# Two changes to the order of VectorE's work in a fused kernel: routing steps moved by a place, weight splits gathered in one tile

## What is computed

```python
logits = x @ w_gate                                  # first layer adds noise, then takes the best two
expert_idx = np.argmax(logits, axis=1)               # second layer: the best one
gate_w = probs[np.arange(N), expert_idx]
for e in range(E):
    xe = x[expert_idx == e]
    out[expert_idx == e] = gate_w * (np.maximum(xe @ w1[e], 0.0) @ w2[e])
```

## Time and profile before

| | us |
|---|---|
| median of 3 runs | 1131.98 |
| lowest and highest | 1128.28 and 1138.9 |
| the profiled execution | 1126.27 |
| its span, first to last instruction | 1124.5 |

### The profile page before, as it was taken

One profiled execution on the slowest core, in us unless ns is written; L12 is line 12 of the kernel. 1 busy time (PEld: TensorE's weight loads), 2 busy tenths in 40 slices (PEclk: granted clock), 3 DMA queues, 4 the chain that ended last, 5 costly groups with the idle time before them and its releaser, 6 DMA issues.

```text
span 1124.5 us, 30641 instructions
## 1 busy us (share of the span) xinstructions
PE 1067.7 (95%) x7894; PEld 998.0 (89%) x7895; DVE 796.0 (71%) x1432; ACT 572.1 (51%) x1233; POOL 488.3 (43%) x530
## 2 busy tenths in 40 slices
PE   3999899999999999999999999999999899999995
PEld 3779799889999899999999899998998888999995
DVE  8998999999588655456566775556678875666652
ACT  2345345545634434455666344446765555655542
POOL 1000455556445444444455344444445544545452
PEclk9998899999999999999999999999999999999998
DMA  8439332342342232445554332335964644543510
GB/s 262 124 106 263 92 117 81 109 120 99 94 115 77 87 98 78 138 148 172 164 154 141 96 92 90 96 108 174 273 200 145 156 113 120 158 130 109 154 44 14
DMA packets 105111, 143.77 MB, mean 128 GB/s; under 512 B 27818, under 2 KB 82413, under 8 KB 104812
## 3 DMA queue, kind: packets, MB, share of 16 engines
q1 hardware_dynamic: 85612, 99.74, 30.5%
q0 software_dynamic: 19456, 43.53, 13.3%
HBM read 111.53 MB, written 35.09 MB: 130 GB/s over the span
## 4 chain that ended last, share of the span: by engine, by line
PE 70%; DVE 12%; issue 8%; DMA 3%; DVEq 2%; ACT 2%; SPq 1%; POOL 0%; ACTq 0%; POOLq 0%
PE ps_y L1937 18%; PE ps_y L1943 9%; PE ps_h L1874 7%; PE ps_h L1878 6%; PE ps_h L1881 6%; PE ps_h L1875 6%; PE ps_h L1862 4%; PE ps_h L1694 3%; DVE h_lo L1086 2%; PE ps_x L1852 2%; PE ps_y L1964 2%; PE ps_x L1851 2%; DVE prod L959 1%; DMA row<-in_moe_w_dram 1%; DVE prod L729 1%
## 5 line engine op out<-in xcount | busy, mean ns | idle before, releaser
L1937 PE MATMUL ps_y<-w_hl,h_hi 128*128 128x400 f32 (+1 forms) x1344 | 370.4, 360 | 2.6 <-DVE y L1106 1.8
L1086 DVE SCALAR_TENSOR_TENSOR h_lo<-ps_h,h_hi 128x512 fp32r<-128x512 f32 x404 | 258.7, 684 | 152.8 <-ACT h_hi L1525 112.4
L598 POOL DMA_INDIRECT row<-x_rows,read_now x200 | 229.3, 1146 | 277.1 <-issue 234.1
L1525 ACT ACTIVATE h_hi<-ps_h 128x512 fp32r<-128x512 f32 x370 | 202.7, 596 | 224.4 <-PE ps_h L1862 137.4
L1943 PE MATMUL ps_y<-w_hl,h_lo 128*128 128x200 f32 (+1 forms) x1344 | 293.5, 259 | 1.1 <-DVE h_lo L1086 1.0
L1937 PEld LDWEIGHTS ps_y<-w_hl,h_hi 128*128 128x128 f32 x1344 | 244.6, 188 | 3.5 <-issue 2.4
L1943 PEld LDWEIGHTS ps_y<-w_hl,h_lo 128*128 128x128 f32 x1344 | 235.6, 191 | 2.1 <-DVE h_lo L1086 2.0
L1874 PE MATMUL ps_h<-xa_hi,w1a_hi 128*128 128x256 f32 x672 | 203.2, 302 | 3.7 <-issue 1.3
L1878 PE MATMUL ps_h<-xa_lo,w1a_hi 128*128 128x256 f32 x672 | 191.1, 284 | 2.8 <-DVE xa_lo L1068 2.6
L1875 PE MATMUL ps_h<-xa_hi,w1a_lo 128*128 128x256 f32 x672 | 189.3, 282 | 0.0
L1881 PE MATMUL ps_h<-xb_hh,w1b_hl 128*128 128x256 f32 x672 | 188.6, 281 | 0.0
(11 more groups left out here) (245 smaller groups left out, 1630.3 us busy)
## 6 DMA issues: line engine op xcount, KB each, us to landing
w_raw<-in_moe_w_dram SPq DMA_DIRECT2D x32, 768.0 KB
w1a_raw<-in_moe_w_dram SPq DMA_DIRECT2D x32, 512.0 KB
w1b_raw<-in_moe_w_dram SPq DMA_DIRECT2D x64, 256.0 KB
x_rows<-tok SPq DMA_DIRECT2D x14, 512.0 KB, 3.3
x_rows<-tok SPq DMA_DIRECT2D x28, 256.0 KB
x_pad<-in_x_dram SPq DMA_DIRECT2D x2, 2688.0 KB, 10.4
row<-x_rows,read_now POOLq DMA_INDIRECT x200
x_pad<-y_rows SPq DMA_DIRECT2D x14, 200.0 KB
```

The source lines that it names most:

```text
L598: pool.indirect_dma_start(out=row[:, buffer, u, 0:XW if p < C else SCALED_W], out_offset=None, in_=x_rows[p], in_offset=bass.IndirectOffse ...
L1086: nc.vector.scalar_tensor_tensor(out=h_lo[:, i * GF:(i + 1) * GF, :], in0=ps_h[:, i, :].rearrange("p (f t) -> p f t", f=GF), scalar=0.0, i ...
L1525: act.activation(h_hi[:, i * GF:(i + 1) * GF, :], ps_h[:, i, :].rearrange("p (f t) -> p f t", f=GF), ACT.Relu).then_inc(h_hi_ready, 1)
L1937: nc.tensor.matmul(first, h_hi[:, i, cols], both_w, start=(i == 0), stop=False)
```

## The change

Two things. In the passes of the second layer (p >= 2) VectorE takes all three low parts of the next expert in the tile in which it takes w1a, and SyncE of the third pass issues all three loads in the expert's first tile. And in the second and third pass routing steps stand elsewhere: `choose_first` part 0 moves from `after_splits` to `before_results` of the same tile; `rank_tokens` moves from the end of tile `SCORE` to `before_splits` of tile `COUNT`; the second half of `count_tiles`, now a function `add_tiles` of eight small instructions, moves from tile `COUNT` into the next one; and `place` part 2 moves from there to `after_splits` of tile `MARK`. The steps of the first pass keep their places.

```diff
@@ -490,14 +490,18 @@
                         load_others(s, nxt)
                     return
                 b0, b1, _ = tile_bounds(sp, p, e)
-                sp.reg_sub(weights_later, b1, 1)
-                sp.reg_alu(weights_later, weights_later, b0 + 2, ALU.min)
+                if p < C:
+                    sp.reg_sub(weights_later, b1, 1)
+                    sp.reg_alu(weights_later, weights_later, b0 + 2, ALU.min)
                 with sp.Fori(b0, b1) as j:
                     side(p, g0, j)
                     with sp.If(j == b0):
                         load_w1_first(s, nxt)
-                    with sp.If(sp.snap(weights_later) == j):
-                        load_others(s, nxt)
+                        if p >= C:
+                            load_others(s, nxt)
+                    if p < C:
+                        with sp.If(sp.snap(weights_later) == j):
+                            load_others(s, nxt)
 
             def experts(p):
 
@@ -842,7 +846,11 @@
                 if part == 0:
                     dve.wait_ge(counts_read, p + 1)
                     count_tiles(p, step, v)
+                    if p < 2:
+                        add_tiles(p, step, v)
                 elif part == 1:
+                    if p >= 2:
+                        add_tiles(p, step, v)
                     give_places(p, step, v)
                 elif part == 2:
                     give_rows(p, step, v)
@@ -859,6 +867,9 @@
 
                 parts(halves[:, :], count_sb[:, 1, :], P)
                 parts(tiles_f[:, :], halves[:, :], SUB)
+
+            def add_tiles(p, step, v):
+
                 step(v.tensor_scalar(expert_base[:, :], tiles_f[:, :], float(SUB), None, ALU.mult))
                 step(v.tensor_tensor(halves[:, :], expert_base[:, :], halves[:, :], ALU.subtract))
                 prefix_sums(v, step, (tiles_f, tiles_end, expert_base, tiles_end), E, lambda buf, lo, hi: buf[:, lo:hi])
@@ -1050,11 +1061,16 @@
                     split_w1a(s, b)
                     e = nc.s_assert_within(s - (p * E + 1), 0, E - 1, skip_runtime_bounds_check_because="the pass has E experts")
                     dve.reg_load(split_1a_at, table[p][0:1, bass.ds(e * 4 + 1, 1)])
-                    dve.reg_sub(split_1b_at, split_1a_at, 1)
-                    dve.reg_alu(split_2_at, split_1b_at, j + 2, ALU.min)
-                    dve.reg_alu(split_1b_at, split_1b_at, j + 1, ALU.min)
-                with dve.If(dve.snap(split_1b_at) == j):
-                    split_w1b(*ahead())
+                    if p < C:
+                        dve.reg_sub(split_1b_at, split_1a_at, 1)
+                        dve.reg_alu(split_2_at, split_1b_at, j + 2, ALU.min)
+                        dve.reg_alu(split_1b_at, split_1b_at, j + 1, ALU.min)
+                    else:
+                        split_w1b(s, b)
+                        dve.reg_mov(split_2_at, j)
+                if p < C:
+                    with dve.If(dve.snap(split_1b_at) == j):
+                        split_w1b(*ahead())
 
             def split_w2_ahead(p, j):
 
@@ -1112,6 +1128,8 @@
                 q = p + 1
                 if p > 0 and j == SCORE[p]:
                     combine_logits(q)
+                if p > 0 and j == COUNT[p]:
+                    rank_tokens(q)
                 if p == 0 and j == SCORE[p] + 3:
                     choose_second(q, 0)
                 if p == 0 and j == COUNT[p] + 1:
@@ -1126,10 +1144,10 @@
                     invert_exps(q)
                 if p == 0 and j == SCORE[p] + 3:
                     choose_second(q, 1)
-                if p > 0 and j == SCORE[p]:
-                    choose_first(q, 0)
                 if p > 0 and j == COUNT[p]:
                     shares(q)
+                if p > 0 and j == MARK[p]:
+                    place(q, 2)
                 if j == LIST[p]:
                     place(q, 3)
 
@@ -1144,14 +1162,14 @@
                 if p == 0 and j == SCORE[p] + 3:
                     rank_tokens(q)
                 if p > 0 and j == SCORE[p]:
+                    choose_first(q, 0)
                     choose_first(q, 1)
-                    rank_tokens(q)
                 if j == COUNT[p]:
                     place(q, 0)
-                if j == COUNT[p] + 1:
-                    if p > 0:
-                        place(q, 1)
+                if p == 0 and j == COUNT[p] + 1:
                     place(q, 2)
+                if p > 0 and j == COUNT[p] + 1:
+                    place(q, 1)
                 if p == 0 and MARK[p] <= j < LIST[p]:
                     mark_some(p, j, 1)
                 if p > 0 and MARK[p] <= j < LIST[p]:
```

## The result

| | before | after |
|---|---|---|
| median of 20 runs each, us | 1133.09 | 1144.24 |
| lowest and highest | 1127.93, 1141.94 | 1137.01, 1152.6 |
| the profiled execution | 1126.27 | 1142.88 |
| its span | 1124.5 | 1141.1 |

The ratio is 1.0098, with a 95% interval of 1.0076 to 1.0119. The prediction said 1131 and no change; the kernel became 11 us slower.

A forecast was written before the change was run, and what follows sets the result against it. TensorE, busy 95% of the span, was taken as the bound, so VectorE edits count only through its stalls. Second pass -1.1, third +1.6, fourth 0: total +0.5 on 1126.27, so 1126.8; median forecast 1131, range 1125 to 1137.5.

The forecast's parts named there:

- Third pass, the loads: w1b and w2 load about 7 us sooner, ending ScalarE's 2.02 us wait for w1b in tile 2; gain 1.6.
- rival E: Loads crowd into one tile beside gathers and scatters, and a late row gather stops TensorE; +4, 1135, chance 0.05.
- The largest term: Third pass, tile 9: all splits and choices pile up on VectorE, count matmuls wait 2.6 us for scans; +2.3 net.
- Second pass: Tile 17, choose_first part 0 moved, -0.8; tile 18, add_tiles leaves, -1.2; tile 20, part 2 ahead of xa_lo, +0.9.
- Third pass, tile 3: TensorE's tile of 11.46 us there shortens as ScalarE no longer waits for w1b; -1.6.
- Tiles 4 to 8: Third pass, experts' first tiles: splits standing together make the next third matmul late by 0.4 in three tiles at most; +1.0.
- Tile 11: Third pass: add_tiles leaves VectorE's tile 10 and the next, a half tile, gains; -1.0.
- Tiles 12 and 13: Third pass: w2 split leaves tile 11, -1.2; part 2 ahead of tile 12's splits, +2.1; y behind it, +0.2.
- Tiles 14 to 16: Third pass: w1b and w2 splits go from VectorE's tile 14 into 13, beside the second block of marks; -0.2.
- Fourth pass: No change, 0, judged by a one-tile expert whose splits already stood back to back with the next tile on time.
- rival B: Slower through the third-pass counts: tile 9's pile, with a late w2 copy, makes them wait 4.6; +5, 1136, chance 0.20.

The follow-up runs named there:

- e9: The changed kernel with two buffers of y and of the list of target rows in the second layer, taken in turn; 1.0027 of the kernel before.
- e5: The changed kernel, but third-pass w1b and w2 loads wait until the scatter of y of the expert's first tile has landed; 1.0040 of the kernel before.
- e8: The changed kernel with nine idle matmuls ahead of the third pass's count matmuls; 1.0070 of the kernel before.
- e2: The changed kernel with second-layer splits and loads put back, so only the routing steps move; 0.9971 of the kernel before.
- e17: The routing moves alone, weight splits and loads as before the change, the same kernel as e2 run again; 0.9977 of the kernel before.
- e3: The changed kernel, but SyncE of the third pass loads w1b and w2 by the old rule, splits still in one tile; 1.0077 of the kernel before.
- e4: The changed kernel with only an eighth of w1b and of w2 loaded in the second layer, splits unchanged; 1.0031 of the kernel before.
- e14: The same kernel as e5, third-pass w1b and w2 held until the scatter has landed, run once more; 1.0083 of the kernel before.

## Why the prediction was wrong

**The step that failed** is that the sum put the cost of the earlier loads at nothing. Third pass, the loads, has a gain of 1.6 and no cost, and crowding stands only as rival E, at 0.05 and with the wrong victim. The text said that a row gather that lands late stops TensorE directly and that none was late. It looked for who waits for a gather and never asked who waits for the scatter. That wait stood in the trace of before, 5.9 us in 3 tiles, and I passed over it because I read the waits of TensorE and not those of VectorE for a DMA. The sum then moved SyncE's loads into tile 0 and asked only who stands behind them in SyncE's queue. The DMA engines as a queue were not walked through, though GpSimd's scatter is issued within 2 us of the new place. The Trainium skill, DMA: Bandwidth & Descriptors, section Issuing engines are not separate DMA queues, was read as speaking against bunching. It says that DMAs started by ScalarE, SyncE and GpSimd interleave on the same 16 DMA engines. The trace agrees, and what follows is the opposite: 1.8 MB of SyncE's are in the way of GpSimd's scatter, y 8.1 us after the issue instead of 3.8. By the profiles the waits of y carry about 40% of what the passes lost (e9); what else the crowded loads hold up stays open.

**The largest term was mis-sized**, with its mechanism right. The count matmuls of the third pass were to wait 2.6 us, net 2.3. They waited 2.42, and the tile grew by 4.5: no term was there for the clock, some 1.7 us of it. (The term itself has a small slip: 865.5 less 862.8 is 2.7, not 2.6.)

**The other steps.** All numbers are lengths of TensorE's tiles, forecast and then measured.
- Second pass: -0.8, -1.2 and +0.9, against -0.9, -1.4 and +1.15. Right, and the third matmul of tile 21 of that pass waits 0.88 for xa_lo as forecast:

```profile
654.01 0.30 PE L1892 MATMUL ps_h<-xa_hi,w1a_hi 128*128 128x256 f32 x1
655.31 0.39 PE L1896 MATMUL ps_h<-xa_lo,w1a_hi 128*128 128x256 f32 x1 [0.88 <-DVE xa_lo L1084]
```

  In e5 and e8, whose part 2 stands as in the change, that tile is only 0.2 longer than before: VectorE waited 0.2 for the last h_hi instead of 0.6. So the term is 0.2 to 1.15 from one execution to the next. The gap behind part 2 is 0.71 us, near the row's 0.74. By the Trainium skill, Advanced Engine Details and Errata, section Control Flow Timing, with its 108 ns for a compare-and-branch, two compares would be 0.2 us, an estimate. The gap of 0.71 is longer, but it holds register instructions too, so it doesn't test that figure.
- Third pass, tile 3: -1.6 against -1.7, right, and outweighed by tile 2, +5.4, forecast 0.
- Tiles 4 to 8: +1.0 against +3.5; three of the eight waits of y for a scatter are here, 4.65 us the longest.
- Tile 11: -1.0 against -1.0. Tiles 12 and 13 together: +1.1 against +0.4. Tiles 14 to 16: -0.2 against +2.2; in tile 14 y, behind marks and w2, makes TensorE wait 1.96.
- Fourth pass: 0 against +4.2. The size isn't settled: e8, whose fourth pass is that of the change, has -0.5 there. I had taken the one-tile expert, where all splits already stood together and the next tile was on time, for the case of all. Where the expert before has more tiles, two splits now stand ahead of xa_lo where one did:

```profile
963.79 0.51 PE L1916 MATMUL ps_h<-w1a_hi,xa_lo 128*128 128x512 f32 x1 [1.13 <-DVE xa_lo L1084]
```

**Right:** that the moved steps nearly cancel (e2, e17), that only few microseconds can be gained, and the place and length of the count wait. **Wrong too:** rival B had the pile but at +5 as the worst; the measured loss of both causes together lay outside every case.

## What to carry to other kernels

When a load moves, walk the DMA engines as one queue of all issuers and ask of each transfer near the new place, a scatter above all, which buffer it holds and who writes that buffer next. Bytes that cost little spread over three tiles can cost microseconds in one. Price a stall of TensorE of two microseconds at its length and again at what the clock loses behind it, 1.7 us here and in some runs 3.4. When a rule is put back to undo a change, compare the times of the transfers too: in e3 the second expert's w1b went out 2.1 us earlier under the old rule. And when an edit takes one wait away, look at the rest of its profile, its end included, before all that it gains is put down to that wait.

## What the runs showed of the hardware

- Stalls of 2.42 us and of 1.6 twice within 5 us were each followed by some 3.4 us at 1.2 GHz. In the count tile the clock fell about 1.4 us after TensorE had started again (872.21; the stretch from 873 has 0.82, as 0.64 us at full speed and the rest at half would give). In e4 the same stall of 2.42 us was followed by some 6.8 us at 1.2 GHz (863.6 to 870.4), and its tile 10 took 16.0 us.
- TensorE stood 1.62 us up to 785.28 in the kernel after, and 2.66 in e9, waiting for nothing that the profile shows, with the half clock behind the latter. Timeline and stretches of e9:

```profile
792.84 0.58 PE L1945 MATMUL ps_h<-xa_hi,w1a_hi 128*128 128x256 f32 x1 [2.66 <-issue]
```

```profile
790.00:792.00 2.00, 0.18 (x2) 0.00 (x0) 0.74 (x2) 1.91 (x6) 0.16 (x1) 1.00 1.05 246
...
793.00:796.00 3.00, 3.00 (x13) 3.00 (x14) 2.30 (x5) 2.15 (x5) 1.99 (x2) 0.50 0.93 338
```

  The DMA list has a packet of an instruction queue of 16 KB, taking about 1.5 us, that starts within 1.7 us ahead of each stall (between 782 and 783 us after, between 789 and 790 in e9), with the engines' share above 1.0. That TensorE's instructions were late through the full DMA engines fits, but was not tried, and the kernel before speaks against it as the whole reason: a packet of the same size and length went through at 784 us there, at a share of 1.01, and TensorE did not stand.
- The same kernel gave 1.0040 and 1.0083 in two runs (e5, e14), so a difference of 4 per mille between kernels that were not run side by side is not to be read.
